# Attention, mixture of experts and MLP on one core: the split of turned queries and keys moves from GpSimd to ScalarE and VectorE

## The reference

```python
scale = 1.0 / np.sqrt(64)                                  # q, k, v: (4, 8, 576, 64), tau = 0.02
scores = scale * np.matmul(q, k.transpose(0, 1, 3, 2))
thresh = np.max(scores, axis=-1, keepdims=True) - tau
scores = np.where(scores >= thresh, scores, -1e9)
attn = np.exp(scores - np.max(scores, axis=-1, keepdims=True))
attn = attn / (np.sum(attn, axis=-1, keepdims=True) + 1e-09)
x = np.matmul(attn, v)                                     # -> (2304, 512)
logits = x @ w_gate + modality_bias[modality_id]           # 8 experts, argmax; gate = its softmax
out[mask] = gate_w[mask, None] * (relu(x[mask] @ w1[e]) @ w2[e])
h = out @ w_in; return (h * sigmoid(1.702 * h)) @ w_out     # d_ff = 2048
```

## Time and profile before

| | us |
|---|---|
| median of 3 runs | 1011.82 (1011.54 to 1012.12) |
| profiled execution, its own time | 1011.9 |
| its span (first to last instruction) | 1010.3 |
| PE (TensorE) busy | 967.1 (96%) |
| DVE (VectorE) busy | 530.6 (53%) |
| ACT (ScalarE) busy | 432.4 (43%) |
| POOL (GpSimd) busy | 286.2 (28%) |

### The profile page before, as it was taken

The page is one execution under the profiler, slowest core; times in us unless marked ns, Lnnn a source line. Parts: engine busy times, 40 slices in busy tenths (PEclk is TensorE's granted clock), DMA queues, the critical chain, the costliest instruction groups (busy, mean ns, idle before and its releaser), DMA issues.

```text
span 1010.3 us, 18677 instructions
## 1 busy us (share of the span) xinstructions
PE 967.1 (96%) x6365; PEld 853.6 (84%) x6366; DVE 530.6 (53%) x1138; ACT 432.4 (43%) x925; POOL 286.2 (28%) x357
## 2 busy tenths in 40 slices
PE   4999999999998899999999999999999999999996
PEld 4777777777676699999999999989999999999995
DVE  5998888999999875411124245522223223222221
ACT  3777787776667713312114254432222222222221
POOL 4766667676666503211112100010010000100101
PEclk8999999999999999999999999999999999999999
DMA  4334343334351506711110633110100100100000
GB/s 88 79 82 94 89 97 91 89 78 91 81 158 45 161 13 208 231 42 42 47 57 21 229 107 101 46 60 1 32 31 0 39 23 23 39 0 0 32 1 32
DMA packets 110669, 70.23 MB, mean 70 GB/s; under 512 B 87161, under 2 KB 95383, under 8 KB 110615
## 3 DMA queue, kind: packets, MB, share of 16 engines
q1 hardware_dynamic: 99959, 53.51, 20.3%
q0 software_dynamic: 4160, 10.51, 3.3%
q10 hardware_dynamic: 6496, 5.54, 1.7%
HBM read 45.68 MB, written 14.70 MB: 60 GB/s over the span
## 4 chain that ended last, share of the span: by engine, by line
PE 76%; DVE 12%; issue 7%; ACT 3%; DVEq 1%; DMA 0%; ACTq 0%; POOL 0%; POOLq 0%
PE s_ps L1842 19%; PE s_ps L1814 13%; PE s_ps L1687 11%; PE pt_ps L1814 6%; DVE probs L835 6%; PE misc L1762 5%; PE o_ps L1762 5%; PE s_ps L1620 5%; PE o_ps L1634 5%; PE pt_ps L1570 4%; DVE scores L1124 2%; ACT probs L1427 1%; PE pt_ps L1679 1%; PE pt_ps L1565 1%; DVE xs L844 1%
## 5 line engine op out<-in xcount | busy, mean ns | idle before, releaser
L1312 DVE TENSOR_TENSOR g<-s_ps,sig 128x384 f32<-128x384 f32 x96 | 53.5, 558 | 277.1 <-ACT sig L1537 277.1
L1537 ACT ACTIVATE sig<-s_ps 128x384 f32<-128x384 f32 x96 | 47.2, 491 | 271.5 <-PE s_ps L1842 271.5
L835 DVE SCALAR_TENSOR_TENSOR probs<-scores,thresh,probs 128x576 f32<-128x576 f32 x144 | 158.5, 1102 | 0.0
L790 POOL DMA_INDIRECT out_dram<-out_sb,table x18 | 17.8, 989 | 417.7 <-ACT out_sb L1512 414.7
L1124 DVE TENSOR_SCALAR_CACHE_REDUCE scores<-s_ps,taus 128x576 f32<-128x576 f32 x144 | 117.6, 817 | 31.2 <-PE s_ps L1620 11.4
L1427 ACT ACTIVATE probs<-scores,row_low 128x576 f32<-128x576 f32 x144 | 113.0, 785 | 45.4 <-DVE scores L1124 44.3
L1570 PE MATMUL pt_ps<-ident,probs 128*128 128x128 f32 x720 | 121.9, 280 | 10.7 <-ACT pT L1335 6.6
L1842 PE MATMUL s_ps<-yT_high,w_in_high 128*128 (+1 forms) x384 | 129.6, 337 | 0.3 <-issue 0.2
L1842 PE MATMUL s_ps<-yT_high,w_in_low 128*128 (+1 forms) x384 | 129.6, 338 | 0.0
L1842 PE MATMUL s_ps<-yT_low,w_in_high 128*128 (+1 forms) x384 | 129.1, 336 | 0.0
L1570 PEld LDWEIGHTS pt_ps<-ident,probs 128*128 128x128 f32 x720 | 83.3, 142 | 41.5 <-issue 25.5
(11 more groups left out here) (273 smaller groups left out, 2221.0 us busy)
## 6 DMA issues: line engine op xcount, KB each, us to landing
w_raw<-in_moe_w_dram SPq DMA_DIRECT2D x24, 512.0 KB, 4.5
yT_dram<-tile_yT ACTq DMA_DIRECT2D x10, 512.0 KB, 3.1
k_parts<-k_swap SPq DMA_DIRECT2D x31, 144.0 KB, 2.3
k_swap<-k_parts SPq DMA_DIRECT2D x31, 144.0 KB, 2.3
x_dram<-xs SPq DMA_DIRECT2D x32, 128.0 KB, 2.3
w_in_raw<-in_moe_w_in_dram SPq DMA_DIRECT2D x4, 1024.0 KB, 5.2
w_out_raw<-in_moe_w_out_dram SPq DMA_DIRECT2D x16, 256.0 KB, 2.7
qk<-in_k_dram SPq DMA_DIRECT2D x30, 128.0 KB, 2.4
```

The lines of the kernel that those rows point to most:

```text
L835: dve.scalar_tensor_tensor(out=probs[:, i % PROB_SLOTS, 0:SEQ], in0=scores[:, i % SCORE_SLOTS], scalar=thresh[:, j, u:u + 1], in1=probs[:, ...
```

## The change

GpSimd's split goes. ScalarE makes the rounded parts (`round_queries`, `round_keys`) in steps 3, 4, 5 and 7 behind the exponential. VectorE makes the rests (`split_rests`), two subtractions in a row per side, in steps 5 (side 0) and 7 (side 1), between the minimum and the mask. Two semaphores (`split_high`, `split_low`) take the place of `parts_ready`. TensorE's nine transposes of queries and keys move into the first five steps of a pair, as (2, 2, 1, 2, 2) tiles, and each group is evicted in its own step. On SP, the key moves of a pair's side 0 and the stores of x come ahead of `load_a`; the moves for pair 0 are issued ahead of the steps, and the loads of `ids`, which stood in front of them, are spread over quads 1 and 2, with the bias operations on VectorE moved from quad 0 to quad 4. One early gather of GpSimd moves from step 13 of the last quad to 11, the other from 11 to 3.

```diff
-        TURN_TILES = {1: (0, 2), 3: (2, 4), 4: (4, 5), 6: (5, 7), 8: (7, 9)}
+        TURN_TILES = [(0, 2), (2, 4), (4, 5), (5, 7), (7, 9)]
...
-                    wait_apart(sp, turned, (quad * 2 + j - 1) * U)
+                    wait_apart(sp, turned, U if isinstance(quad, int) and quad * 2 + j == 2 else (quad * 2 + j - 2) * U + TPB)
...
-            def swap_keys(quad, j, side):
-                split = (quad * 2 + j) * 8 + side * 4 - 4
+            def move_keys(quad, j, side):
+                cols, pair = K_COLS[side], quad * 2 + j
+                wait_apart(sp, split_high, (pair * 2 + side) * 2)
                 sp.dma_start(k_parts[j][TOP, cols].bitcast(F32), k_swap[j][BOTTOM, cols].bitcast(F32)).then_inc(k_swapped[side], 16)
-                wait_apart(sp, parts_ready, split + 2)
+                wait_apart(sp, split_low, (pair * 2 + side) * 2 - 1)
                 sp.dma_start(k_swap[j][TOP, cols].bitcast(F32), k_parts[j][BOTTOM, cols].bitcast(F32)).then_inc(k_swapped[side], 16)
...
                     if on(pair, 0, PAIRS):
                         load_v(quad, j)
+                    if on(pair, 2, PAIRS + 2):
+                        store_x(quad - 1, j)
+                    if on(pair, 0, PAIRS - 1):
+                        move_keys(quad + j, 1 - j, 0)
+                    if w1_pass:
+                        load_w1(first_expert_of(sp), 0, range(2, DB))
                     if on(pair, 0, PAIRS - 2):
                         load_a(quad + 1, j)
-                    if on(pair, 0, PAIRS - 1):
-                        swap_keys(quad + j, 1 - j, 0)
...
+                    if quad in (1, 2):
+                        load_ids(quad - 1, j)
...
+            move_keys(0, 0, 1)
             step(0)
...
-                pool.tensor_copy(k_swap[j][BOTTOM, cols], qkT_raw[BOTTOM, cols]).then_inc(parts_ready, 1)
-                pool.tensor_tensor(k_parts[j][BOTTOM, cols], qkT_raw[BOTTOM, cols], k_swap[j][BOTTOM, cols].bitcast(F32),
-                                   ALU.subtract).then_inc(parts_ready, 1)
...
+            def split_rests(pair, j, side):
+                cols = K_COLS[side]
+                wait(dve, split_high, (pair * 2 + side) * 2)
+                dve.tensor_tensor(k_parts[j][BOTTOM, cols], qkT_raw[BOTTOM, cols], k_swap[j][BOTTOM, cols].bitcast(F32), ALU.subtract
+                                  ).then_inc(split_low, 1)
+                dve.tensor_tensor(q_parts[j][BOTTOM, Q_COLS[side]], qkT_raw[TOP, cols], q_parts[j][TOP, Q_COLS[side]].bitcast(F32),
+                                  ALU.subtract).then_inc(split_low, 1)
...
+                    if u in (5, 7) and on(pair, 0, PAIRS - 1):
+                        split_rests(pair + 1, 1 - j, 0 if u == 5 else 1)
...
+                act.copy(q_parts[j][TOP, Q_COLS[side]], qkT_raw[TOP, K_COLS[side]]).then_inc(split_high, 1)
...
+                act.copy(k_swap[j][BOTTOM, K_COLS[side]], qkT_raw[BOTTOM, K_COLS[side]]).then_inc(split_high, 1)
...
+                    if u in (3, 4, 5, 7) and on(pair, 0, PAIRS - 1):
+                        side = 0 if u < 5 else 1
+                        if u in (3, 5):
+                            wait_apart(act, turned_copied, pair * U + U + (TAIL - 1 if side == 0 else TPB))
+                            round_queries(1 - j, side)
+                        else:
+                            round_keys(1 - j, side)
...
-                    mm = transpose_qk(1 - j, tu, pt_ps[:, QK_AT + TURN_SLOT[tu]])
+                if with_qk and tu < TPB:
+                    first, end = TURN_TILES[tu]
+                    for tile in range(first, end):
+                        mm = transpose_qk(1 - j, tile, pt_ps[:, QK_AT + tile - first])
```

More of the change, by code:

```diff
@@ L566, in early_part, with load_ids @@
                     sp.wait_ge(turned, UNITS)
-                    sp.wait_ge(parts_ready, PAIRS * 8 - 4)
+                    sp.wait_ge(split_high, (PAIRS * 2 - 1) * 2)
+                    sp.wait_ge(split_low, (PAIRS * 2 - 1) * 2)
                     sp.wait_ge(order_stored, 16)
                     load_w2(first_expert_of(sp), 0)
+            def load_ids(bp, part):
+                at = bp * U
+                id_words = modality_id.bitcast(I32).rearrange("(b s w) -> b s w", b=BATCH, w=2)[:, :, 0]
+                ids_of = id_words[2 * bp + part]
+                rows, tail, cols = ((slice(0, LAST), SEQ - LAST, slice(at, at + TAIL)) if part == 0 else
+                                    (slice(LAST, P), SEQ - LAST, slice(at + TPB, at + U)))
+                sp.dma_start(ids[:, cols], ids_of[0:SEQ - LAST].rearrange("(t p) -> p t", p=P),
+                             allow_slow_non_contiguous=True).then_inc(routing_loaded, 16)
+                sp.dma_start(ids[rows, at + TAIL:at + TPB], ids_of[tail:].rearrange("(t p) -> p t", t=1),
+                             allow_slow_non_contiguous=True).then_inc(routing_loaded, 16)
             def first_expert_of(sp):
@@ L577, in step @@
                     pair = quad * 2 + j
+                    w1_pass = isinstance(quad, int) and (quad, j) == (QUADS - 2, 1)
                     if on(pair, 0, PAIRS - 2):
                         load_b(quad + 1, j)
-                    if on(pair, 0, PAIRS):
-                        swap_keys(quad, j, 1)
+                    if on(pair, 1, PAIRS):
+                        move_keys(quad, j, 1)
                     if isinstance(quad, int):
                         early_part(quad, j)
-                    if isinstance(quad, int) and (quad, j) == (QUADS - 2, 1):
+                    if w1_pass:
                         sp.wait_ge(first_expert_ready, 1)
@@ L736, in step @@
                     pair = quad * 2 + j
-                    if isinstance(quad, int) and quad == QUADS - 1 and i in (11, 13):
+                    if isinstance(quad, int) and quad == QUADS - 1 and i in (3, 11):
                         pool.wait_ge(x_stored[0], PAIRS // 2 * 4 * 16)
@@ L1338, in copy_turned @@
                     act.copy(extra, extra_ps[0:extra.shape[0], 0:extra.shape[1]]).then_inc(extra_copied, 1)
-                last = None
                 if with_probs:
                     last = act.copy(pT[:, TAIL, v * P:(v + 1) * P], pt_ps[:, TAIL])
-                if with_qk and tu in TURN_TILES:
-                    if tu in (1, TAIL):
-                        wait(act, parts_ready, pair * 8 + (0 if tu == 1 else 4))
-                    if isinstance(pair, int) and pair == 0 and tu == 1:
+                if with_qk and tu < TPB:
+                    if tu in (0, 2):
+                        wait(act, split_low, (pair * 2 + (0 if tu == 0 else 1)) * 2)
+                    if isinstance(pair, int) and pair == 0 and tu == 0:
                         act.wait_ge(first_queries, 2)
@@ L1610, in score @@
                     side = 0 if u == 0 else 1
-                    wait(pe, parts_ready, pair * 8 + side * 4)
+                    wait(pe, split_low, (pair * 2 + side) * 2)
                     wait(pe, k_swapped[side], (pair + side) * 2 * 16)
```

72 lines of the change are left out of this document (14 added, 58 removed).

## The result

The changed kernel took 1015.99 us (median of 7 runs, 1013.86 to 1017.39) against 1012.12 (7 runs) for the kernel before, in the same series: a ratio of 1.0038, 95% interval 1.0026 to 1.0050. It is 0.4% slower; 1014.5 was forecast. The profiled execution took 1015.67 us with a span of 1014.1, 3.8 us more than before.

The account below looks back on a forecast made before the run. VectorE was taken to bound the attention loop. Start -6.9, pair 1 +1.7, loop +9.7 and unrolled pairs -1.9 summed to +2.6 us, for a forecast of 1014.5 us, range 1006 to 1020.

Parts of the forecast that it names:

- GpSimd's share falls away: Attention stage: VectorE's masks are no longer stretched by GpSimd's split; gain 12.3 + 22.8 + 2.0 + 4.8 us.
- Four subtractions, 3.37 us a pair: VectorE in attention: four 64x576 subtractions cost 3.37 us per pair, as changes of partition half lose the overlap.
- overlap rival: VectorE's subtractions overlap with their neighbours, so 2.7 us per pair and 1005 us in all; chance 0.12.
- Side costs 0.3 a pair: Two costs of VectorE's new order in attention, 0.15 us per pair each, together 0.3.
- (a): Without long masks, the value product between units 1 and 2 on TensorE comes into sight: 0.15 us per pair (0 to 0.4).
- (b): GpSimd's addition may slip between three VectorE operations in a row: 0.15 us per pair (0 to 0.3).
- Roundings on ScalarE hidden: ScalarE in attention: four roundings per pair, 2.3 us in 19.4, fit its idle time and are charged nothing.
- first rival: ScalarE becomes the bound, its pT copy late behind a rounding in steps 4 to 6: 1021 us; chance 0.16.
- The start, -6.9: Earlier key moves end TensorE's stall, so minimum 11 comes at 33.7 instead of 40.55: -6.9 us (-5 to -8.5).
- Free, as long as those 2.3 us last: SP's queue: load_a, behind stores and key moves, lands at 7.5 us and is wanted at 9.8, at no cost.
- this rival: load_a comes late, 1 us beyond its 2.3 of slack in each pair: 1028 us; chance 0.05.

Follow-up runs that it names:

- e4: The changed kernel, but in pairs 2 to 11 both rests of a half replaced by two subtractions on the lower partitions only: 1010.51 us, ratio 0.9995.
- e6: The changed kernel with the rests on GpSimd in steps 5 and 7 and load_a issued before the stores and key moves: 995.92 us, ratio 0.9841.
- e2: The changed kernel with load_a issued before the stores of x and the key moves: 1011.88 us, ratio 1.0001 to the kernel before.
- e5: The kernel of e2 with one more 64x576 copy on ScalarE in step 3 of pairs 0 to 10: 1013.59 us, ratio 1.002.
- e7: The kernel of e2 with one VectorE subtraction of 128x576 per half instead of two of 64x576, and three moves per half: 995.08 us, ratio 0.9837.
- e3: The changed kernel with the four rests of a pair on GpSimd, in steps 5 and 7, instead of VectorE: 1041.23 us, ratio 1.0302.

## Why the prediction came out as it did

**The mechanism was right:** the start's gain is given back in the loop, by subtractions that cost VectorE more than GpSimd's disturbance did (e4, e6). That the total came within 1.5 us of the forecast is in part luck: the late loads, forecast at nothing, cost 4 us, and the rest of the sum came out 2.6 us too high.

- *GpSimd's share falls away*: right. Masks of 814 ns everywhere. That the long masks of before lie beside GpSimd's subtractions is not the whole of it: in the unrolled pairs some lie behind a rounding copy (last section).
- *Four subtractions, 3.37 us a pair*: right, 3.4: the minima of units 6 and 8 come 3.50 us behind the ones in front of them, where a usual step takes 1.81. e4 shows the cause, the changes of half. The overlap rival (2.7) falls.
- *Side costs 0.3 a pair*: (a), the value product coming into sight, is there as 0.38 of wait for `s_ps` at one minimum a pair, 0.14 over the usual 0.24. (b), GpSimd's addition slipping between, is not there. In 14 pairs that is 2.1 us too much; it is the term that was mis-sized. The unrolled pairs gave 0.9 and pair 1 some 0.5 beyond it, for which no run has the cause. So e2, without the late loads, equals the kernel before, where 2.6 above it was forecast.
- *Roundings on ScalarE hidden*: supported. A third one costs 0.14 of its 0.57 (e5), with the keys of unit 7 as the tight place. The first rival did not come.
- *The start, -6.9*: -5.9. Minimum 4 came at 18.43 for 18.0, and the step to minimum 11 took 2.54 instead of 1.72. That is side cost (a), at the start 0.8 us instead of 0.15: VectorE's steps are 1.72 there and 1.81 in the loop, so it reaches the value product sooner. TensorE did wait 0.81 for `qk` at 28.09, but e2, without that wait, gains only 0.1 from minimum 4 to 11.
- *SP: "Free, as long as those 2.3 us last"*: this step failed. The last load of a pair was to land 7.5 us after unit 5's minimum and be wanted at 9.8. In the pair of the rows above, that minimum is at 104.91. The last load landed at 112.13, 7.2 later, as reckoned, but TensorE transposes the new tiles at 112.25, 7.3 later: it runs a unit ahead of VectorE, having two buffers of scores, and does so before the score that I counted from. The slack is not 2.3 but about nothing. Where an issue on SP takes 1.16 instead of 0.52 us (65.57) it is negative. I gave this rival 0.05, at 1 us a pair. It came, in some pairs: 4 us in all (e2), half of it in the one pair in which the clock fell behind the wait. Whether it is also why the changed kernel's runs spread over 3.5 us and e2's over 1.8 is not shown: e7's, with the loads of e2, spread over 3.0.

## What to carry to other kernels

When one transfer is moved behind another's wait, reckon its slack from the instruction that reads it on the engine that runs ahead, not from the pace of the slowest engine. A short wait of TensorE can cost more than itself: look at the granted clock behind it (1.6 us a pair in e3). Before work is moved to the engine that bounds a stage, count its operations and the partitions they start on: one operation over 128 partitions costs as much as one over 64, and two that change half cost 1.68 us where one costs 0.67. A split change should be timed part by part: here the start alone gave 0.3%, and the rest gave back more than that.
